# Attention and two dense layers on one core: the third head's k in its own buffer, and four moves of order around the end of the bias stage

## The reference

```
q, k, v: 4 sequences x 8 heads x 576 x 64, float32
scores = q @ k.T / sqrt(64) + bias[head]          # 576 x 576
x[i, j] = log1p(|i - j|) / log1p(max(i, 1))
bias[i, j, head] = relu(x * w1 + b1) @ w2         # 32 hidden units, the same for all sequences
attn = softmax(scores);  a = attn @ v             # heads joined: 2304 x 512
h = a @ moe_w_in;  z = (h - tanh(h)) @ moe_w_out  # 512 -> 2048 -> 512
g = z @ w_gate;  out = (g * sigmoid(g) * (z @ w_val)) @ moe2_w_out   # 512 -> 1536 -> 512
```

## Time and profile before

| | |
|---|---|
| median of 3 runs | 1225.61 us (1223.7 to 1226.31) |
| profiled execution, its own time | 1224.13 us |
| its span, first to last instruction | 1222.2 us |
| TensorE busy | 1178.2 us |
| VectorE, ScalarE, GpSimd busy | 595.8, 569.6, 531.5 us |
| mean granted TensorE clock | 0.997 |
| transfers | 125.46 MB, mean 103 GB/s |

### The profile page before, as it was taken

One profiled execution on the slowest core, in us unless ns is written; L12 is line 12 of the kernel. 1 busy time (PEld: TensorE's weight loads), 2 busy tenths in 40 slices (PEclk: granted clock), 3 DMA queues, 4 the chain that ended last, 5 costly groups with the idle time before them and its releaser, 6 DMA issues.

```text
span 1222.2 us, 20183 instructions
## 1 busy us (share of the span) xinstructions
PE 1178.2 (96%) x7320; PEld 1080.2 (88%) x7320; DVE 595.8 (49%) x1377; ACT 569.6 (47%) x1163; POOL 531.5 (43%) x584
## 2 busy tenths in 40 slices
PE   6769899999999999999999999999999999999998
PEld 2346699999999998999899999999999999999998
DVE  8957777756565657666666534321211212122111
ACT  7968577655565556556555554422211222121212
POOL 0048677765666657777878522111111111111111
PEclk9989999999999999999999999999999999999999
DMA  6878464444343434455555344100000000000000
GB/s 198 277 238 260 141 190 139 126 128 119 111 143 113 116 97 141 132 145 135 154 135 140 123 135 149 52 26 27 27 1 27 26 26 26 1 26 1 26 1 26
DMA packets 77763, 125.46 MB, mean 103 GB/s; under 512 B 17120, under 2 KB 40672, under 8 KB 77664
## 3 DMA queue, kind: packets, MB, share of 16 engines
q1 hardware_dynamic: 77664, 124.16, 34.2%
HBM read 104.07 MB, written 20.05 MB: 102 GB/s over the span
## 4 chain that ended last, share of the span: by engine, by line
PE 83%; DVE 10%; issue 3%; ACT 2%; POOL 1%; DMA 1%; SPq 0%; DVEq 0%; POOLq 0%; ACTq 0%
PE ps_y L1484 14%; PE ps_h L1465 13%; PE ps_s L1586 12%; PE ps_y L1597 12%; PE ps_h L1586 6%; PE ps_pt L1586 6%; PE ps_s L1382 6%; PE ps_pt L1436 5%; PE ps_pt L1401 5%; DVE feat L1090 4%; PE ps_pt L1465 1%; DVE prob L1125 1%; DVE fr L1175 1%; DVE wbuf L1141 1%; ACT prob L804 1%
## 5 line engine op out<-in xcount | busy, mean ns | idle before, releaser
L739 POOL TENSOR_TENSOR fr<-tanh_b,fr 128x384 fp32r<-128x384 f32 x72 | 73.2, 1017 | 377.9 <-ACT fr L1017 377.9
L1484 PE MATMUL ps_y<-fr,wbuf 128*128 128x384 f32 x1152 | 230.4, 337 | 0.0
L1465 PE MATMUL ps_h<-fr,wbuf 128*128 128x384 f32 x1056 | 206.1, 338 | 1.5 <-DVE fr L1175 1.1
L1484 PEld LDWEIGHTS ps_y<-fr,wbuf 128*128 128x128 f32 x1152 | 198.2, 188 | 0.8 <-POOL fr L681 0.8
L1465 PEld LDWEIGHTS ps_h<-fr,wbuf 128*128 128x128 f32 x1056 | 181.6, 188 | 3.3 <-issue 1.8
L804 ACT ACTIVATE prob<-prob,negmax 128x576 f32<-128x576 f32 (+1 forms) x160 | 124.0, 775 | 115.2 <-DVE negmax L1125 114.7
L676 POOL TENSOR_SCALAR prob<-prob,rowinv 128x576 f32<-128x576 f32 (+1 forms) x160 | 127.6, 799 | 110.2 <-DVE rowinv L1136 110.2
L1597 PE MATMUL ps_y<-wbuf,fr 128*128 128x512 f32 x648 | 161.1, 393 | 0.0
L681 POOL TENSOR_TENSOR fr<-g_b,fr 128x384 fp32r<-128x384 f32 x96 | 100.6, 1048 | 115.8 <-ACT fr L835 115.8
L1597 PEld LDWEIGHTS ps_y<-wbuf,fr 128*128 128x128 f32 x648 | 120.5, 188 | 22.1
L1125 DVE CUSTOM_DVE_ANT_0 prob<-ps_s,biasb 128x576 f32<-128x576 f32 (+1 forms) x147 | 110.0, 748 | 13.7 <-PE ps_s L1382 12.5
(11 more groups left out here) (134 smaller groups left out, 1946.0 us busy)
## 6 DMA issues: line engine op xcount, KB each, us to landing
biasb<-bias_scratch SPq DMA_DIRECT2D x64, 288.0 KB, 3.2
raw<-k_t SPq DMA_DIRECT2D x59, 288.0 KB, 3.1
biasb<-bias_scratch SPq DMA_DIRECT2D x64, 216.0 KB, 2.8
bias_scratch<-w_raw SPq DMA_DIRECT2D x72, 144.0 KB, 3.2
biasb<-bias_scratch SPq DMA_DIRECT2D x64, 144.0 KB, 2.9
w_raw<-w_chunks SPq DMA_DIRECT2D x16, 512.0 KB, 5.2
prob<-w_chunks SPq DMA_DIRECT2D x8, 768.0 KB, 4.8
raw<-v_p SPq DMA_DIRECT2D x36, 160.0 KB, 2.3
```

Of the source, the lines that this page charges most:

```text
L1465: mm = eng.matmul(hidden_bank(u, c)[:, 0:TOK], w[:, cols], x[:, d, :], start=d == 0 and i == 0, stop=d == KC - 1 and i == 2)
L1484: mm = eng.matmul(ps_y[:, d, 0:TOK], w[:, cols], g[c % 2], start=c == 0 and i == 0, stop=c == C1 - 1 and i == 2)
```

## The change

Five edits, in the order of the diff:

1. k of head 2 gets a buffer of its own, `k_raw_two`, in a region (`w1_raw[4]`) behind three of the places of `bias_ev`, and a semaphore, `d_k_two`. It is loaded in the bias stage, right after q of head 2, ahead of the stores of rounds 29 and 31. `K_SUM` no longer counts it.
2. The loads of bias tiles 4 and 5 no longer stand among the last stores. All stores come first, then the loads of tiles 4, 5 and 6 in a row.
3. `split_k` is cut in two, `k_high` and `k_low`.
4. The high parts of k of heads 0 and 1 are made as soon as 12 of the 36 rounds have left TensorE. Their low parts wait for the last feature, as before.
5. The exponential of one column, and with it the load of the exponential's table, goes ahead of the last `evacuate`.

```diff
-    k_sum[own] += 16
+    k_sum[own] += 0 if hd.n == 2 else 16
...
+        k_raw_two = w1_raw[4][:, :, :, :, :].rearrange("p c i s n -> p (c i s n)")[:, 6 * S:7 * S]
...
+            def load_k_two():
+                eng.dma_start(k_raw_two, k_t[HEADS[2].seq * H + HEADS[2].h, :, :]).then_inc(d_k_two, 16)
...
             for rnd in range(1, NQUAD, 2):
-                if rnd >= NQUAD - 4:
-                    load_bias(BR + (rnd - (NQUAD - 4)) // 2)
                 store_bias(rnd)
...
                     load_q(HEADS[2])
-            load_k(HEADS[2])
-            load_bias(BR + 2)
+                    load_k_two()
+            for tile in range(BR, BR + 3):
+                load_bias(tile)
...
+            def k_source(hd):
+                if hd.n == 2:
+                    return k_raw_two
+                return k_raw_even if own_raw(hd) else k_raw
+
+            def k_high(hd, moe):
+                if hd.n == 2:
+                    eng.wait_ge(d_k_two, 16)
+                else:
+                    eng.wait_ge(d_k_even if own_raw(hd) else d_k, K_SUM[hd.n])
                 _, hi, lo = operands(hd, moe)
                 wait(eng, e_score, preparing(hd, moe))
                 hold(eng)
-                src = k_raw_even if own_raw(hd) else k_raw
-                eng.tensor_scalar(hi, src, 1.0, 1.0, ALU.mult, ALU.mult).then_inc(p_khi, 1)
+                eng.tensor_scalar(hi, k_source(hd), 1.0, 1.0, ALU.mult, ALU.mult).then_inc(p_khi, 1)
+
+            def k_low(hd, moe):
+                _, hi, lo = operands(hd, moe)
                 eng.wait_ge(p_khi, hd.n + 1)
-                eng.tensor_tensor(lo, src, hi.bitcast(F32), ALU.subtract).then_inc(p_klo, 1)
+                eng.tensor_tensor(lo, k_source(hd), hi.bitcast(F32), ALU.subtract).then_inc(p_klo, 1)
...
+            eng.wait_ge(e_feat, GQ)
+            k_high(HEADS[0], [])
+            k_high(HEADS[1], [])
             eng.wait_ge(v_feat, feat_done(NQUAD - 1, V_FEAT))
-            split_k(HEADS[0], [])
-            split_k(HEADS[1], [])
+            k_low(HEADS[0], [])
+            k_low(HEADS[1], [])
...
+            eng.activation(spare, b1_col, ACT.Exp)
             evacuate(NQUAD - 1)
-            eng.activation(spare, b1_col, ACT.Exp)
```

More of the change, by code:

```diff
@@ L225, in attention_layers_kernel @@
         d_q, d_k, d_v, d_v_odd = sem("d_q"), sem("d_k"), sem("d_v"), sem("d_v_odd")
-        d_q_even, d_k_even = sem("d_q_even"), sem("d_k_even")
+        d_q_even, d_k_even, d_k_two = sem("d_q_even"), sem("d_k_even"), sem("d_k_two")
         d_bias = [sem(f"d_bias{i}") for i in range(BR)]
@@ L648, in _ @@
                               pattern=[[-1, P]], channel_multiplier=1).then_inc(pool_tab, 1)
-            def split_k(hd, moe):
-                eng.wait_ge(d_k_even if own_raw(hd) else d_k, K_SUM[hd.n])
+            def k_source(hd):
[7 more added lines that the diff above has]
+                    eng.wait_ge(d_k_even if own_raw(hd) else d_k, K_SUM[hd.n])
                 _, hi, lo = operands(hd, moe)
@@ L656, in split_k @@
                 hold(eng)
-                src = k_raw_even if own_raw(hd) else k_raw
-                eng.tensor_scalar(hi, src, 1.0, 1.0, ALU.mult, ALU.mult).then_inc(p_khi, 1)
+                eng.tensor_scalar(hi, k_source(hd), 1.0, 1.0, ALU.mult, ALU.mult).then_inc(p_khi, 1)
+            def k_low(hd, moe):
+                _, hi, lo = operands(hd, moe)
                 eng.wait_ge(p_khi, hd.n + 1)
-                eng.tensor_tensor(lo, src, hi.bitcast(F32), ALU.subtract).then_inc(p_klo, 1)
+                eng.tensor_tensor(lo, k_source(hd), hi.bitcast(F32), ALU.subtract).then_inc(p_klo, 1)
+            def split_k(hd, moe):
+                k_high(hd, moe)
+                k_low(hd, moe)
             def split_v(hd):
```

## The result

The changed kernel takes 1220.59 us (median of 8 runs, 1219.89 to 1222.07) against 1224.49 (8 runs, 1223.51 to 1226.31): ratio 0.9968, 95% interval 0.9959 to 0.9978, so 3.9 us or 0.32% faster. That the time of 1220.4 came out so near is luck: the median of the kernel before fell by 1.1 us with five more runs. The profiled execution took 1222.07 us (span 1220.2), the longest of the eight; it is only 2.0 us shorter in its span than that of before. The executions' mean granted clocks go from 0.997 to 1.000 (0.997 and 1222.07 us, 1.000 and 1220.18 us at the ends).

The account below looks back on a forecast made before the run. TensorE was busy 1178.2 of 1222.2 us, so only the remaining 44 us or its slowed clock could be won. Terms: -6.2 (k, clock, later bias load) + 1.0 (features delayed) = -5.2, 1220.4 us from 1225.61; range 1217.4 to 1223.6.

Parts of the forecast that it names:

- What bounds the kernel; k early: End of bias stage: GpSimd's 5.2 us wait for head 2's k goes; its subtraction ends at 75.5, not 81.3.
- Stores ahead of the bias loads: the new wait: VectorE at tile 4: its bias, issued behind the stores, lands at 74.65, a new wait of about 1.7 us.
- The clock: TensorE over head 2's stretch: clock stays up, gaps near 1 us each; if it falls, 1.8 us are lost again.
- A falling clock: Sign at TensorE, 67 to 88 us: granted clock 1.00 expected; the prediction is wrong if the clock still falls.
- First two k rounded inside the stage: GpSimd among VectorE's features: gain hidden by the bias wait, features delayed 1.0 us; ends nothing and 1.34.
- The table: Exponential's table load ahead of the last bias copy: worth nothing within the bias wait's slack, up to 0.5 us without it.
- Rival 2, the transfers set the pace: Queues from 66.0 us: only some 275 GB/s come, 2.1 us more; gain 3.1, 1222.5 us; chance 0.19.
- Rival 3: Tile 4 and loads behind it land after 6 us, 1.34 lost on VectorE: no change, about 1224 us; chance 0.10.
- From there the shift reaches the end: Behind 84 us of the span: everything waits for TensorE or its feeders, so the 5.2 us shift should reach the end.

Follow-up runs that it names:

- k alone: Kernel before with only head 2's k loaded early into its own buffer; 1220.52 us against 1224.26, ratio 0.9963.
- six last, late rounding: Changed kernel with six stores (rounds 25 to 35) behind loads of heads 5 to 7, first two k rounded after the last feature; 1218.52 us, ratio 0.9945.
- two stores last: Changed kernel with the stores of rounds 33 and 35 moved behind all loads of head 7's turn; 1217.92 us against 1225.24, ratio 0.9947.
- six stores last: Changed kernel with the six stores of rounds 25 to 35 moved behind the loads of heads 5, 6 and 7; 1218.86 us against 1225.24, ratio 0.9947.
- before, six last: Kernel before, none of the five edits, six stores moved out of the bias stage, head 2's k right behind tile 4's bias; 1218.47 us against 1225.24, ratio 0.9944.
- the kernel with the fillers: Changed kernel with 18 unread identity matmuls ahead of head 2's first scores in TensorE's gap; 1220.36 us against 1224.58, ratio 0.9965.
- the stores behind: Changed kernel with the last two groups of stores behind the bias loads of tiles 4 to 6; 1221.77 us against 1224.58, ratio 0.9975.
- the stores spread: Changed kernel with the stores of rounds 33 and 35 behind head 1's and head 2's loads, wait in head 3's turn; 1220.24 us against 1224.58, ratio 0.9962.
- the kernel with late rounding: Changed kernel with the k of heads 0 and 1 rounded after the last feature again; 1220.38 us against 1224.26, ratio 0.9962.

## Why the prediction was right, and where it was not

*What bounds the kernel; k early.* Right. GpSimd's wait for k is gone, and its low part ended at 76.3 where 75.5 was forecast; the features, 0.7 us later, were a term of their own.

*Stores ahead of the bias loads: the new wait.* The mechanism was right, the size was not; this is the term that was mis-sized. The prediction had SyncE finish the stores at 70.3 and issue tile 4's second load at 70.95. It was 72.65 and 73.15. 0.9 us of the 2.3 is the later start of the stores (62.9 for 62.0, most of it the features' delay, charged elsewhere), and 1.4 the time of the sixteen issues: 9.71 us, while I had added up 4.12, 1.98 and 2.20, thus 8.30. It is not that every issue became slower. Fourteen took 0.42 to 0.60 us; the fourth took 1.04 and the eleventh 1.74:

```profile
64.35 1.04 SPq L487 DMA_DIRECT2D bias_scratch<-w_raw  x1
...
68.54 1.74 SPq L487 DMA_DIRECT2D bias_scratch<-w_raw  x1
```

In the five other profiles with sixteen stores in a row they took 9.04 to 9.28 us, the longest issue 1.2 to 1.5. What holds such an issue up is not shown. The load then took 3.82 us, as forecast (3.7). VectorE's wait became 3.88 us, and 2.4 to 3.5 in the other profiles, not about 1.7.

*The clock.* "I take the clock to stay up: the gaps of TensorE left are near 1 us each." This failed: the gap was 2.99 us, and the granted clock went to 0.67 and 0.65. A falling clock was one of the signs by which the prediction called itself wrong, and that sign came. The premise was not safe either: in two profiles with gaps near 1.1 us only (*k alone*, *six last, late rounding*) the clock fell too, in three (*two* and *six stores last*, *before, six last*) it stayed; what decides it, no run shows. The price it had been given, 1.8 us, was 2.2 here (6.73 against 4.50) and 2.4 by the kernel with the fillers. Together: 2.35 us won at head 2's third scores in place of 5.2. In the median over executions 3.9 were won: the profiled one was the longest of the eight, and the others show a higher mean clock, 0.998 to 1.000 against 0.997. So the step that failed in size is the new wait, taken as 1.7 us, with the clock that was to stay up behind it.

*First two k rounded inside the stage.* Forecast 1.0 us of delay, with 1.34 as its upper end, measured 0.7: two features took 0.92 and 0.91 us instead of 0.57; that its gain is hidden is borne out as far as the intervals go. *The table.* Forecast at nothing; the run that undid it won 0.7 to 1.0 us less, in overlapping intervals. Open.

*Rival 2, the transfers set the pace,* with a chance of 0.19, was what decided. It did not act as one rate over the whole stretch. It acted through waits that move with the stores: to k before, to tile 4's bias in the change, to head 3's k and q and tile 7's bias with the stores behind, to heads 4 and 5 with the stores spread, and in *two stores last* nowhere. Rival 3 had the mechanism in its words, "the wait only changed its name", though not the size. The 3.9 us lie between the forecast and rival 2 (3.1, or 3.4 if the low clock stays); how much of the rest is the longer wait and how much the clock, in the median of the runs, is not shown.

*"From there the shift reaches the end."* Right for the change: 2.6 us at head 0's product, 2.0 at the end of the span. Not so for a bigger gain: the spread stores lost 1.8 of 6.3 us within seven heads.

## What to carry to other kernels

Where a load is late, look at what stands ahead of it in its queue before moving the load. If that is a store, ask who reads it first: here 3.5 MB were on their way by 75 us that no score uses before 447 us, and moving them won more (6.8 us) than five edits on the side that waited (3.9). A long row of issues needs a term for single slow ones: in each of six profiles the row of sixteen took 0.7 to 1.4 us more than the sum of shorter rows. And a gap of TensorE is priced with the low clock that may follow, even a gap near 1 us.

## What the runs showed of the hardware that was not expected

Single issues on SyncE's queue take far longer than the rest. Of sixteen stores of 144 KB in a row, at a DMA share of 0.9, fourteen took 0.42 to 0.60 us and two 1.04 and 1.74. The eight stores of the earlier trace rows at 61.53 took 4.12 us in all, at a share of 0.95 from 60 to 66 us, so the share alone does not make them slow.

TensorE's clock fell or stayed behind nearly the same work. From 67 to 76.4 us TensorE ran the same instructions at the same times, to 0.03 us, in *k alone* and *before, six last*, with a last gap of 1.1 us in both. The next stretch took 5.95 us in one and 4.51 in the other, with granted clocks of 0.71 and 1.00.

GpSimd's two roundings among unbroken features took 1.01 and 0.87 us instead of 0.67, and two features 0.92 and 0.91 instead of 0.57; the whole chain lost 0.7 us.

In four of the fourteen profiled executions, of four different kernels, the bias rounds at 12 to 16 us ran slowly: 2.15 us for sixteen matmuls that took 1.21 in the others, while the window's granted clock read 1.00 in both. It moved all that followed by 1.05 us. The first line is from the kernel with late rounding, the second from the kernel before:

```profile
11.89 2.15 PE L1385 MATMUL ps_s<-feat,prob 128*32 128x288 f32 x16 [0.73 <-DVE feat L1108]
```

```profile
11.88 1.21 PE L1367 MATMUL ps_s<-feat,prob 128*32 128x288 f32 x16 [0.96 <-DVE feat L1090]
```

Its cause was not looked for.
